# Outputs of a chunked linear attention formed with v and the state stationary from round 5 on, then turned back

## The reference

```python
for t in range(S):                                   # B=2, H=8, S=768, D=48
    kt, vt, rt, wt = k[:, :, t], v[:, :, t], r[:, :, t], w[:, :, t]
    cur = einsum('bhd,bhe->bhde', u[None] * kt, vt)
    y[:, :, t] = einsum('bhd,bhde->bhe', rt, state + cur)
    state = wt[:, :, :, None] * state + einsum('bhd,bhe->bhde', kt, vt)
# x = y as (B, S, H*D) = (2, 768, 384)
h = gelu(x @ w_in); u, v = halves(h)                 # 384 -> 1024, two halves of 512
x = x + (u * (w_sg @ layernorm(v) * g + b_sg)) @ w_out
u = x + (relu(x.T @ w_tok1) @ w_tok2).T
out = u + relu(u @ w_ch1) @ w_ch2                    # 384 -> 1536 -> 384
```

## Time and profile before

| | |
|---|---|
| median of 3 runs | 405.75 us (405.57 to 406.07) |
| the profiled execution | 405.78 us, span 404.3 us |
| TensorE busy | 392.1 us, 97% of the span |
| VectorE, ScalarE, GpSimd busy | 47%, 28%, 40% of the span |
| share of the last chain on TensorE | 90% |
| rounds 5 to 11 | 46.0 to about 133 us of the span |

### The profile page before, as it was taken

The page is one execution under the profiler, slowest core; times in us unless marked ns, Lnnn a source line. Parts: engine busy times, 40 slices in busy tenths (PEclk is TensorE's granted clock), DMA queues, the critical chain, the costliest instruction groups (busy, mean ns, idle before and its releaser), DMA issues.

```text
span 404.3 us, 6836 instructions
## 1 busy us (share of the span) xinstructions
PE 392.1 (97%) x2638; PEld 377.0 (93%) x2638; DVE 188.4 (47%) x397; ACT 114.3 (28%) x224; POOL 161.6 (40%) x180
## 2 busy tenths in 40 slices
PE   5999899999999999999999999999999999999997
PEld 4788788898899999899999999999999999999996
DVE  5889988678664452314443736350132123103301
ACT  3257526565412020673001212340021012002200
POOL 5764787684425662585899970000000000000000
PEclk9999999999999999999999999999999999999999
DMA  9999598553110202002113310000100100000001
GB/s 146 129 234 227 97 207 198 118 99 92 46 41 2 78 2 78 2 1 79 39 49 109 117 42 0 2 0 21 39 2 0 41 20 2 19 21 19 2 19 39
DMA packets 60129, 25.03 MB, mean 62 GB/s; under 512 B 51136, under 2 KB 58176, under 8 KB 60096
## 3 DMA queue, kind: packets, MB, share of 16 engines
q1 hardware_dynamic: 60096, 24.58, 27.8%
HBM read 22.22 MB, written 2.36 MB: 61 GB/s over the span
## 4 chain that ended last, share of the span: by engine, by line
PE 90%; DVE 5%; issue 2%; POOL 1%; ACT 1%; DVEq 0%; POOLq 0%; ACTq 0%
PE bank L1062 25%; PE bank L1064 24%; PE bank L1063 24%; PE bank L1152 4%; PE bank L1076 3%; PE bank L1148 3%; DVE suf L846 2%; PE bank L1187 2%; PE bank L1113 2%; PE bank L1205 1%; PE bank L1120 1%; PE bank L1131 1%; DVE pre L858 1%; POOL rp L555 1%; DVE am L882 1%
## 5 line engine op out<-in xcount | busy, mean ns | idle before, releaser
L754 ACT ACTIVATE ha_hi<-bank 128x384 fp32r<-128x384 f32 x48 | 23.6, 492 | 113.1 <-PE bank L1064 113.1
L989 DVE SCALAR_TENSOR_TENSOR ha_lo<-bank,ha_hi 128x384 fp32r<-128x384 f32 x48 | 26.8, 558 | 50.2 <-ACT ha_hi L754 50.2
L1062 PE MATMUL bank<-c_hi,ha_lo 128*128 128x384 f32 x144 | 48.2, 335 | 0.0
L1064 PE MATMUL bank<-c_hi,ha_hi 128*128 128x384 f32 x144 | 48.1, 334 | 0.0
L1064 PE MATMUL bank<-u2T_hi,c_hi 128*128 128x384 f32 x144 | 48.1, 334 | 0.0
L1063 PE MATMUL bank<-c_lo,ha_hi 128*128 128x384 f32 x144 | 48.1, 334 | 0.0
L1062 PE MATMUL bank<-u2T_hi,c_lo 128*128 128x384 f32 x144 | 48.1, 334 | 0.0
L1063 PE MATMUL bank<-u2T_lo,c_hi 128*128 128x384 f32 x144 | 48.1, 334 | 0.0
L994 DVE TENSOR_TENSOR x<-bank,x 128x384 f32<-128x384 f32 x12 | 6.7, 558 | 65.3 <-PE bank L1064 65.3
L1062 PE MATMUL bank<-sg_hi,z_lo 128*128 128x384 f32 x96 | 32.5, 338 | 0.0
L1064 PE MATMUL bank<-sg_hi,z_hi 128*128 128x384 f32 x96 | 32.1, 334 | 0.0
(11 more groups left out here) (142 smaller groups left out, 886.2 us busy)
## 6 DMA issues: line engine op xcount, KB each, us to landing
raw<-in_moe_w_ch SPq DMA_DIRECT2D x12, 384.0 KB, 3.1
kc<-in_k SPq DMA_DIRECT2D x12, 192.0 KB, 4.4
rc<-in_r SPq DMA_DIRECT2D x12, 192.0 KB, 5.0
vn<-in_v SPq DMA_DIRECT2D x12, 192.0 KB, 5.0
raw<-in_moe_w_sg SPq DMA_DIRECT2D x6, 384.0 KB, 4.0
out<-x SPq DMA_DIRECT2D x12, 192.0 KB, 1.9
raw<-in_moe_w_in SPq DMA_DIRECT2D x4, 384.0 KB, 4.8
raw<-in_moe_w_tok SPq DMA_DIRECT2D x4, 384.0 KB, 3.3
```

The source lines that it names most:

```text
L754: sc.activation(ha[0][:, i, :], bank[:, 0:HALF], ACT.Relu).then_inc(act_out, 1)
L989: ve.scalar_tensor_tensor(ha[1][:, i, :], bank[:, 0:HALF], 0.0, ha[0][:, i, :].bitcast(F32), ALU.max, ALU.subtract).then_inc(dve_out, 1)
L1062: te.matmul(dst, left[1], right[0], start=first, stop=False)
L1064: return te.matmul(dst, left[0], right[0], start=False, stop=last)
```

## The change

From round 5 on the outputs are formed the other way round: `outputs_across` takes the state and v as the stationary operands and r and the masked scores as the moving ones, so that the result is turned (112 partitions of heads by 128 tokens, in bank `bs[0]`). ScalarE copies it (`take_yT`, into `yT`), and TensorE turns it back with four transposes (`turn_y`, into bank `by`, heads 64 columns apart) behind the jobs of slot 1. VectorE's `y_tile` and `x_tile` move behind its slot 1. `sbd` has 64 columns a head instead of 48 and lies elsewhere. In rounds 5 and 11 k isn't turned back and not copied.

```diff
-    sbd = put("sbd", [PART, 2, NP, 2 * D])
+    yT = put("yT", [PART, NP, PART])
+    sbd = put("sbd", [PART, 2, NP, 2, HP])
@@ ScalarE
+            def take_yT(n):
+                act.wait_ge(av_done, n + 1)
+                if n > YR:
+                    act.wait_ge(y_turned, n - YR)
+                sc.copy(yT[0:QP, :, :], pairs(bs[0])[0:QP, :, :]).then_inc(yt_copied, 1)
-                take_k(n)
+                if n % NC < NC - 1:
+                    take_k(n)
...
+                if n >= YR:
+                    take_yT(n)
                 for piece in high.get(n, ()):
                     split_high(*piece)
                 for job in slot_jobs(n, 1):
@@ VectorE
-                y_tile(n)
-                if n >= YR:
-                    x_tile(n)
+                if n < YR:
+                    y_tile(n)
                 if n + 2 < NCH:
                     backward(n + 2)
                 take_slot(n, 1)
+                if n >= YR:
+                    y_tile(n)
+                    x_tile(n)
@@ TensorE
+            def outputs_across(n):
+                yb = bs[0]
+                wait_ring(pe, v_in, n)
+                inner = n % NC > 0
+                if inner:
+                    pe.wait_ge(sbd_done, 2 * states(n - 1))
+                pe.wait_ge(masked, 2 * (n + 1))
+                for p in range(NP):
+                    if inner:
+                        te.matmul(yb[0:QP, tile(p)], sbd[0:QP, n % 2, p, :, :].rearrange("c i q -> c (i q)")[:, 0:QP],
+                                  rp[0:QP, n % 2, p, :], start=True, stop=False)
+                    for i in range(2):
+                        h = 2 * p + i
+                        wide = HP if i == 0 else D
+                        ins = te.matmul(yb[HP * i:HP * i + wide, tile(p)], vn[:, n % VR, D * h:D * h + wide], am[:, h, :],
+                                        start=not inner, stop=True)
+                ins.then_inc(av_done, 1)
+            def turn_y(n):
+                pe.wait_ge(yt_copied, n - YR + 1)
...
+                for p in range(NP):
+                    ins = te.transpose(by[:, PART * p:PART * p + QP], yT[0:QP, p, :], ident[0:QP, 0:QP])
+                ins.then_inc(y_turned, 1)
...
                 scores(n)
-                turn_kp(n)
+                if n % NC < NC - 1:
+                    turn_kp(n)
...
-                outputs(n)
+                if n < YR:
+                    outputs(n)
+                else:
+                    outputs_across(n)
...
+                if n >= YR:
+                    turn_y(n)
                 if n % NC < NC - 1:
                     state_products(n)
```

More of the change, by code:

```diff
@@ L235, in build @@
         kn_copied, rt_copied, sbd_done, checked = sem("kn_copied"), sem("rt_copied"), sem("sbd_done"), sem("checked")
-        table_in = sem("table_in")
+        table_in, yt_copied, y_turned = sem("table_in"), sem("yt_copied"), sem("y_turned")
         rp_done, rk_done, rku_done, base_done, flagged = (sem("rp_done"), sem("rk_done"), sem("rku_done"),
@@ L312, in build, with heads_of, heads @@
         bw, b1, b2, bs, by, bc = ps[0], ps[1], ps[2], ps[3:5], ps[5], ps[7]
+        def heads_of(bank):
+            return bank[:, :].rearrange("t (h q) -> t h q", h=H)[:, :, 0:D]
+        def heads(t):
+            return t.rearrange("t (h d) -> t h d", h=H)
         def pairs(bank, n=PART):
@@ L676, in take_k @@
             def take_k(n):
-                act.wait_ge(kn_turned, n + 1)
-                if n and n % NC:
+                act.wait_ge(kn_turned, states(n))
+                if n:
                     act.wait_ge(ds_done, states(n - 1))
@@ L695, in take_state @@
                 q = (n + 1) % 2
-                sc.copy(sbd[0:D, q, :, 0:D], st[0:D, :, :]).then_inc(sbd_done, 1)
-                sc.copy(sbd[HP:QP, q, :, D:2 * D], st[HP:QP, :, :]).then_inc(sbd_done, 1)
+                sc.copy(sbd[0:D, q, :, 0, 0:D], st[0:D, :, :]).then_inc(sbd_done, 1)
+                sc.copy(sbd[HP:QP, q, :, 1, 0:D], st[HP:QP, :, :]).then_inc(sbd_done, 1)
+            def take_yT(n):
[3 more added lines that the diff above has]
+                sc.copy(yT[0:QP, :, :], pairs(bs[0])[0:QP, :, :]).then_inc(yt_copied, 1)
             def check_range(i):
@@ L785, in split_high @@
                     act.wait_ge(st_done, states(NCH - 1))
+                    act.wait_ge(av_done, NCH)
                 hi = split_target(name, i, 0)
                 sc.copy(hi, raw_view(piece, hi)).then_inc(w_hi_act, 1)
-            high = {4: [("w_in", 2), ("w_in", 3)], 5: [("w_in", 0)], 6: [("w_in", 1)], 11: [("w_out", 0), ("w_out", 1)]}
+            high = {5: [("w_in", 0)], 6: [("w_in", 1)], 11: [("w_out", 0), ("w_out", 1)]}
             act.wait_ge(v_consts, V_CONSTS)
@@ L806, in _ @@
                     normal(b, i)
+                if n == YR - 1:
+                    split_high("w_in", 2)
+                    split_high("w_in", 3)
+                if n >= YR:
+                    take_yT(n)
                 for piece in high.get(n, ()):
@@ L865, in scale_k @@
                     dve.wait_ge(qk_done, n)
-                    dve.wait_ge(kn_turned, n)
+                    dve.wait_ge(kn_turned, states(n - 1))
                 ve.tensor_tensor(kp[0:QP, :, :], pairs(b1)[0:QP, :, :], suf[0:QP, n % 2, :, 1:PART + 1], ALU.mult
@@ L898, in y_tile @@
             def y_tile(n):
-                dve.wait_ge(av_done, n + 1)
                 dve.wait_ge(base_done, n + 1)
-                dst = x[:, 0, n, :] if n < YR else by[:, 0:C]
-                ve.tensor_tensor(dst, by[:, 0:C], yt[:, n % BR, :], ALU.add).then_inc(y_done, 1)
+                if n < YR:
+                    dve.wait_ge(av_done, n + 1)
+                    ve.tensor_tensor(x[:, 0, n, :], by[:, 0:C], yt[:, n % BR, :], ALU.add).then_inc(y_done, 1)
+                else:
+                    dve.wait_ge(y_turned, n - YR + 1)
+                    ve.tensor_tensor(heads_of(by), heads_of(by), heads(yt[:, n % BR, :]), ALU.add).then_inc(y_done, 1)
             def x_tile(n):
@@ L909, in x_tile @@
                 dve.wait_ge(y_done, n + 1)
-                dst = x[:, n // NC, n % NC, :]
-                ve.scalar_tensor_tensor(dst, by[:, 0:C], okm[:, 1:2], dst, ALU.min, ALU.max).then_inc(x_out, 1)
+                dst = heads(x[:, n // NC, n % NC, :])
+                ve.scalar_tensor_tensor(dst, heads_of(by), okm[:, 1:2], dst, ALU.min, ALU.max).then_inc(x_out, 1)
             def mark_range():
@@ L1100, in turn_r @@
                 if n:
-                    pe.wait_ge(kn_copied, n)
+                    pe.wait_ge(kn_copied, states(n - 1))
+                    pe.wait_ge(rt_copied, n)
                 turn(b2, rc[:, n % KR, :, :]).then_inc(rt_done, 1)
@@ L1109, in scores @@
                     pe.wait_ge(masked, 2 * n)
+                if n > YR:
+                    pe.wait_ge(yt_copied, n - YR)
                 for p in range(NP):
@@ L1125, in state_products @@
                 wait_ring(pe, v_in, n)
-                pe.wait_ge(kn_copied, n + 1)
+                pe.wait_ge(kn_copied, states(n))
                 pe.wait_ge(kp_done, n + 2)
@@ L1137, in outputs @@
                 wait_ring(pe, v_in, n)
-                if n > YR:
-                    pe.wait_ge(x_out, n - YR)
-                elif n:
+                if n:
                     pe.wait_ge(y_done, n)
@@ L1147, in outputs @@
                     if inner:
-                        te.matmul(by[:, 2 * D * p:2 * D * (p + 1)], rp[0:QP, n % 2, p, :], sbd[0:QP, n % 2, p, :],
+                        te.matmul(by[:, 2 * D * p:2 * D * (p + 1)], rp[0:QP, n % 2, p, :], sbd[0:QP, n % 2, p, :, 0:D],
                                   start=True, stop=False)
@@ L1154, in outputs @@
                 ins.then_inc(av_done, 1)
+            def outputs_across(n):
[17 more added lines that the diff above has]
+                pe.wait_ge(yt_copied, n - YR + 1)
+                if n > YR:
+                    pe.wait_ge(x_out, n - YR)
+                else:
+                    pe.wait_ge(y_done, n)
+                for p in range(NP):
+                    ins = te.transpose(by[:, PART * p:PART * p + QP], yT[0:QP, p, :], ident[0:QP, 0:QP])
+                ins.then_inc(y_turned, 1)
             def sum_range():
@@ L1172, in free_bank @@
                     pe.wait_ge(x_out, NCH - YR)
-                    pe.wait_ge(kn_copied, NCH)
+                    pe.wait_ge(kn_copied, states(NCH - 1))
             def product(kind, b, i):
```

## The result

The changed kernel takes 408.56 us (median of 6 runs, 408.53 to 408.63) against 405.73 us: 1.0069 times as long, with a 95% interval of 1.0056 to 1.0082. The prediction was 408.2 us. The profiled execution took 408.60 us, with a span of 407.1 us, 2.8 us more than before.

What follows compares the result with a forecast made beforehand. TensorE, busy for 97% of the span, bounds the kernel. Its own sum of +4.15 us, waits of -1.4 and -0.4 and a start of +0.05 give +2.4 on 405.78: 408.2 us, range 404.2 to 410.3.

Steps and rivals of the forecast that it cites:

- The switch: Outputs on TensorE: changing between whole array and column tiles makes a pair 0.77 us, +0.40 us in each of six rounds.
- rival of cheap switches: Outputs on TensorE: loads are prepared across the switch, a pair takes 0.44 us, 401.3 us in all; chance 0.11.
- chains that don't overlap: Outputs on TensorE: the two column chains run in turn at 128 moving columns, +6.2 us, 414.4; chance 0.02.
- Turning back: turn_y on TensorE: four transposes, 0.38 us in each of seven rounds, +2.7 us; a late copy yT would add waiting.
- Kp: Rounds 5 and 11 on TensorE: of the transposes left out only round 11 gives its four back, -0.35 us.
- The waits: TensorE's waits: -0.7 us in each of rounds 8 and 9 before w_sg transposes, -0.4 in round 5, +0.05 at the start.
- the wait for the Gelu: Round 5: TensorE's 0.36 us wait for ScalarE's Gelu is covered by turn_y, -0.4 us.
- the later state cost nothing: VectorE's state comes 1.2 us later, taken at nothing; uncovered up to 0.5 us a round in rounds 7 to 10.
- the room that it listed: Before outputs(9) need the state: a product of slot 2, the scores, two groups of transposes and slot 0.
- Round 6: Outputs of round 6, which has no state: 1.14 us on TensorE against 1.72 us, -0.6 us.
- Round 5: Round 5 as a whole: +0.38 us, from the prediction's own terms for outputs, turn_y and the Gelu wait.
- the start: Start of the kernel: the larger memset of sbd delays TensorE's first matmul by 0 to 0.25 us, counted as 0.05.

Runs made afterwards that it cites:

- e1: The changed kernel with the four state products of an output round first and the eight v products behind them: 404.09 us.
- e2: The changed kernel with each state product cut into two column tiles (64 and 48 columns), like the v products: 404.19 us.
- e4: The kernel before, with k of rounds 5 and 11 not turned back and not copied: 405.38 us.
- e3: The kernel before, with VectorE's y_tile and x_tile behind its slot 1 from round 5 on: 405.11 us.
- e7: e6 with w turned behind the first product of slot 1 in round 6: 402.91 us.
- e6: e1 with ScalarE's second v normalization in round 8 behind slot 1, and VectorE's slot 0 low parts ahead of scaling k in round 5: 403.30 us.

## Why the prediction was right, step by step

- **The switch.** 0.77 us a pair was forecast and 0.76 measured, 3.02 us a round and 2.97 measured (87.86 to 90.84 in round 8). Its decisive step, that a price read from long groups with a wait on their first load also holds where tiles alternate every two records, was shown by e1 and e2 from two sides: the same records without the inner switches take 1.99 us, eight more records in one kind of tile 1.91 us (2.42 and 2.43 us counted from the transposes of r). The rival of cheap switches falls with them, and so does that of chains that don't overlap. The rule of the Trainium skill (TensorEngine Tiling (Array Packing), Key Properties) that a change of mode drains TensorE agrees with the trace, at 0.20 us from start to start where 0.11 is the rule; what is loaded in the open behind it brings a switch to some 0.165 us (e1). The swap that the Trainium skill recommends (TensorEngine Tiling (Array Packing), Performance Considerations) pays too, once the inner switches are gone, but an output round does not fall to about half: 2.0 us against 2.6. Only the v products of a pair halve (four records in 0.22 us in e2, 86.93 to 87.15, against 0.41 us); the state product hardly changes (0.26 us, now 0.22).
- **Turning back.** 0.38 us each were forecast. In round 8 turn_y starts at 93.78 and takes 0.55 us to the end of its last matmul, 0.27 of which is that one matmul: three starts 0.1 us apart; rounds 7 and 10, which have no wait, got longer by 0.78 and 0.74 us in all, 0.36 of them by the outputs. No copy yT was late in the changed kernel. In e1 ScalarE's queue was, in round 8.
- **Kp.** Only round 11 gives its transposes back; e4 shows it alone.
- **The waits.** In rounds 8 and 9 about 0.65 us each came back, forecast 0.7; in round 5 the wait for the Gelu went, covering turn_y. Which part of the change does this was read only half right: VectorE's order alone gets half of it back (e3). That the later state cost nothing, as the prediction took it, was in part luck: the room that it listed was not enough, turn_y, which it did not count there, made up for it, and 0.09 us was left.
- **Round 6, the one term that was wrong.** The prediction had -0.6 us for its outputs, and the runs show -0.1 (1.50 + 0.09 us against 1.72): it counted TensorE's saving and did not ask whether turn_w behind it was free. The new wait is some 0.5 us for VectorE's `pre`; e7 gets 0.4 us back by putting a product in front. This is the difference between 408.2 and 408.56. Round 5 was 0.1 us better than forecast and the start 0.1 us worse, which is within what executions differ.

## What to carry to other kernels

Count the changes of tile kind on TensorE as instructions of their own: here each cost as much as one and a half f32 records of 128 columns, and they turned a swap that is worth 0.6 us a round into a loss of 0.4 us, before the 0.38 us for turning the result back. Put matmuls of one kind behind each other, or give the odd one the others' shape even if that makes more of them. And when TensorE's queue gets shorter, look at each of its next waits as if it were new: of the 5.9 us that e1 took from the queue a quarter waited elsewhere, and where two engines are late at the same moment, moving one can show nothing (e6).

## What the runs showed of the hardware

That a switch costs the same 0.20 us from start to start in both directions and for row and column tiles was in the rows before. New was that column tiles keep their double rate when products of 112 rows and of 128 rows take turns (e2: eight records of a pair in 0.44 us, where the whole array takes 0.11 us a record), and that a state product of 64 and 48 columns in two tiles is no slower than one of 112 columns on the whole array (0.22 us each, and 2.43 against 2.42 us from the transposes of r to those of w).
